# Reordered maxima and wider routing operands in an attention and mixture-of-experts kernel

## The chip, the core and the metric

The kernel runs on one core of a Trainium2 chip. The time is the device time of one execution in microseconds (us); of several executions the median counts. Before the change it is 771.11 us (three runs, 770.67 to 771.77).

A core has a matrix engine (TensorE, PE in the profile; its weight loads are PEld), VectorE (DVE), ScalarE (ACT), GpSimd (POOL), and SyncE (SP), which issues the transfers here. Each engine takes its own instructions strictly in order; between engines there are only semaphores. SBUF is the working memory, PSUM the memory that TensorE writes its products to.

## What is computed

Three layers in a row, all in float32. Inputs have batch 4, 8 heads, 576 tokens of head width 64; the later layers see 2304 rows of 512.

```python
# attention, block-causal with blocks of 64
scores = scale * q @ k.T
scores = where(block_i >= block_j, scores, -1e9)
attn = exp(scores - max(scores)); attn /= sum(attn) + 1e-9
x = attn @ v
# channel mix; x_prev is x one token earlier
xk = mu_k * x + (1 - mu_k) * x_prev;  xr = mu_r * x + (1 - mu_r) * x_prev
x = sigmoid(xr @ w_r) * (relu(xk @ w_k) ** 2 @ w_v)
# one of 8 experts for each token
logits = x @ w_gate
for each token s of a batch row:
    fresh = argmax(logits[s])
    e = fresh if s == 0 or sigmoid(x[s] @ w_local) < 0.5 else previous e
    out[s] = softmax(logits[s])[e] * (relu(x[s] @ w1[e]) @ w2[e])
```

## The kernel before

Products of float32 operands are mostly made of "rounded" parts: an operand is split in a high part (`hi`, the value as float32r) and the rest (`lo`), and the product is the sum of hi x hi, hi x lo and lo x hi. Much of VectorE's, ScalarE's and GpSimd's work is this splitting.

**Attention (0 to about 197 us).** Each of the 32 heads (4 batches of 8) is one round of a loop over `i`, and every engine has that loop written out by hand; the order of the calls in it is the order on the engine. A head has five query tiles of 128 rows, the last with 64 (tiles 0 to 4). The softmax needs each row's maximum before the scores that go to exp are made. Therefore the work is spread over heads: in round `i`

- TensorE makes the masked scores of head `i` in five pieces (`head_scores`, L732 and L733), the products from which the maxima of head `i+2` are read (`head_max`, L707, and L710 for tile 4), the transpose that turns the maxima of head `i+1` into a row (`head_row`, L718), and the value products of head `i` (`head_pv_split`, L774 and L779, and `head_pv_late`, L787 to L789; `head_pv`, L753, in the last four heads). `head_max` has four groups: group 0 is tiles 0 and 1, groups 1, 2, 3 are tiles 2, 3, 4. Groups 0 to 2 wait only at the first of them; group 3 writes to banks of the first two groups and so waits for their maxima (`max_reduced`, count 4i+2).
- VectorE reads the maxima (`head_reduce`, L1380, and L1383 for tile 4), copies the row of L718 (`copy_row`, L1391), casts q and k of head `i+3` (`cast_hi`, L1402), makes the low parts of q (`split_q_lo`, L1407), of the probabilities (`split_p`, L1491), in even rounds of v (`split_v`, L1483 and L1485), and of one piece of the next layer's weights (`split_wm_lo`, L1415, from round 5 on), and inverts the row sums of head `i-1` (`invert`, L1396).
- ScalarE does the exps (L1151), copies of the results out of PSUM (L1175) and the high parts.
- GpSimd makes the low part of k of head `i+3` (`split_k`, L531), which waits for `split_q_lo` of the same head, and multiplies the output of head `i-3` by its inverted sums (`normalise`, L540), which waits for a transfer.

`head_row` of head `i+1` stands in round `i` and waits for all four groups of maxima of that head, of which VectorE takes the last at the end of round `i-1`.

**Channel mix (about 197 to 476 us).** Six steps of 384 tokens, TensorE full with products (`mlp_step`).

**Routing and experts.** While the last two steps run, the routing of the first 12 groups of 128 tokens is worked out (`pre_route`), the remaining 6 follow at 476 to 484 us. Scans along the tokens are done on VectorE, first within a group of 128 (`local`), then over groups (`carry`); transposes and small products on TensorE bring them to the layout needed (`send_local` L853 and L854, `send_carry` L859, `rank_pre` L876, `rank_base` L1025). After that TensorE runs the expert products, 128 tokens a tile.

Of the kernel before, what the change touches and what calls it, by code (L numbers as in the profile page):

```python
# [5 lines left out]
F32 = mybir.dt.float32  # L6
# [3 lines left out]
R32 = mybir.dt.float32r  # L10
# [6 lines left out]
def attention_moe_program(nc, qkT, v, mu_k, mu_r, w_k, w_v, w_r, w_gate9, w1, w2, out):  # L17
# [36 lines left out]
    with ExitStack() as ctx:  # L54
# [138 lines left out]
        keep = place("x", "keep", [G, NG])  # L193
        fresh = place("x", "fresh", [G, NG])
        holds = place("x", "holds", [NG, G])
        local = place("x", "local", [NG, G])
        unset = place("x", "unset", [1, NG])
        carry = place("x", "carry", [1, NG + 2], R32)
        code = r3("code", 1)
        onehot_any = r3("onehot_any", NE, NPRE)  # L200
        onehot_pre = place("x", "onehot_pre", [G, NE, NPRE], R32)
# [3 lines left out]
        cnt_pre = place("x", "cnt_pre", [P, NE])  # L205
        ones_r = place("x", "ones_r", [G, P], R32)
        behind_r = place("x", "behind_r", [G, G], R32)
        base_pre_r = place("x", "base_pre_r", [1, NE, NPRE], R32)
        base_fin_r = place("x", "base_fin_r", [1, NE, NFIN], R32)
        most = place("x", "most", [P, 1])  # L210
        ties = place("x", "ties", [P, NE])
        first_code = place("x", "first_code", [P, 1])
# [477 lines left out]
        def _(pe):  # L690
# [107 lines left out]
            for i in range(NHEAD):  # L798
                ahead = i + 2 < NHEAD
                head_scores(i, (0, 1))  # L800
                if i + 1 < NHEAD:
                    head_row(i + 1)
                if ahead:
                    head_max(i + 2, (0,))
                head_scores(i, (2, 3, 4))
                if ahead:
                    head_max(i + 2, (1,))
                if i < NSPLIT:
                    head_pv_split(i, (0, 1))
                    head_max(i + 2, (2,))  # L810
                    head_pv_split(i, (2, 3, 4, 5))
                    head_max(i + 2, (3,))
                    head_pv_late(i)
                    continue
                head_pv(i, (0, 1))
                if ahead:
                    head_max(i + 2, (2,))
                head_pv(i, (2, 3))
                if ahead:
                    head_max(i + 2, (3,))  # L820
                head_pv(i, (4, 5, 6))
# [28 lines left out]
            def send_local(n, bank, dve_sem, pe_sem):  # L850

                pe.wait_ge(dve_sem, 2)
                nc.tensor.transpose(ps[0:1, bank, P:P + n], local[0:n, G - 1:G], ident[0:n, 0:n])  # L853
                nc.tensor.transpose(ps[0:G, bank, 0:n], local[0:n, :], ident[0:n, 0:n]).then_inc(pe_sem, 1)  # L854

            def send_carry(n, dve_sem, pe_sem):

                pe.wait_ge(dve_sem, 3)
                mm(ps[0:G, 2, 2 * P:2 * P + n], ones_r[0:1, :], carry[:, 0:n], start=True, stop=True).then_inc(pe_sem, 1)  # L859

            def flat(a):

                return a[:, :, :].rearrange("p e g -> p (e g)")
# [6 lines left out]
            def rank_pre():  # L870

                pe.wait_ge(pre_dve, 5)
                dst = ps[0:G, 2, 0:NE * NPRE]
                mm(dst, ones_r[:, :], flat(incl_pre), start=True, stop=False)
                mm(dst, behind_r[:, :], flat(onehot_pre), start=False, stop=False)
                mm(dst, ones_r[0:1, :], flat(base_pre_r), start=False, stop=True).then_inc(pre_pe, 1)  # L876

            def slot_0_pre():

# [142 lines left out]
            def rank_base():  # L1022

                mm(ranks, ones_r[:, :], incl_pre[:, :, NPRE - 1:NPRE].to_broadcast([G, NE, NFIN]), start=True, stop=False)
                mm(ranks, ones_r[0:1, :], flat(base_fin_r), start=False, stop=False)  # L1025

            def rank_fin():

# [340 lines left out]
        def _(dve):  # L1369
# [124 lines left out]
            for i in range(NHEAD):  # L1494
                if i + 1 < NHEAD:
                    copy_row(i + 1)
                if i + 2 < NHEAD:
                    head_reduce(i + 2, 0)
                if i % 2 == 0 and i < NSPLIT:
                    split_v(i // 2)  # L1500
                if WFIRST < i:
                    split_wm_lo(i - 1 - WFIRST)
                if i + NBUF < NHEAD:
                    cast_hi(i + NBUF)
                if i < NSPLIT:
                    split_p(i)
                if i + NBUF < NHEAD:
                    split_q_lo(i + NBUF)
                if i + 2 < NHEAD:
                    head_reduce(i + 2, 1)  # L1510
                    head_reduce(i + 2, 2)
                if i:
                    invert(i - 1)
                if i + 2 < NHEAD:
                    head_reduce(i + 2, 3)
                if i == NHEAD - 3:
                    dve.wait_ge(k_split, NHEAD)
                    dve.wait_ge(q_split, NHEAD)
                if i in (NHEAD - 3, NHEAD - 1):
                    for c in range(2):  # L1520
                        sum_xm(0, 0, c + (i == NHEAD - 1) * 2)
                if i == NHEAD - 2:
                    for c in range(2):
                        xm0_lo(c)
# [5 lines left out]
            def link(ins):  # L1530

                links[0] += 1
                ins.then_inc(chain, 1)
                dve.wait_ge(chain, links[0])
# [100 lines left out]
            def carry_scan(n, bank, pe_sem, dve_sem):  # L1635

                dve.wait_ge(pe_sem, 2)
                link(vec.tensor_scalar(unset[:, 0:n], ps[0:1, bank, P:P + n], 0.0, None, ALU.is_equal))
                vec.tensor_tensor_scan(carry[:, 1:n + 1], unset[:, 0:n], ps[0:1, bank, P:P + n], 0.0,
                                       ALU.mult, ALU.add).then_inc(dve_sem, 1)  # L1640

            def codes(gs, bank, pe_sem):
# [50 lines left out]
            def pre_route(d):  # L1693

                if d == 0:
                    dve.wait_ge(const_done, 3)
                    dve.wait_ge(logits_read, NPRE // GPS)
                    vec.memset(carry[:, 0:1].bitcast(F32), 0.0)
                    vec.tensor_copy(ones_r[:, :], ones_g[:, :])
                    vec.tensor_copy(behind_r[:, :], behind[:, :])  # L1700
                    vec.tensor_copy(base_pre_r[:, :, :], base_pre[:, :, :])
                    vec.tensor_copy(base_fin_r[:, :, :], base_fin[:, :, :])
                    vec.memset(val_1[:, :, 1].bitcast(F32), 0.0)
                    group_tops(pre, pre_dve)
                if d == 1:
                    local_scan(NPRE, pre_pe, pre_dve)
                    carry_scan(NPRE, 3, pre_pe, pre_dve)
                if d == 2:
                    codes(pre, 3, pre_pe)
                    link(vec.tensor_tensor(onehot_any[:, :, :], revs[:, :, pre], over_e(code, pre), ALU.is_equal))  # L1710
                    vec.tensor_reduce(cnt_pre[:, :], onehot_any[:, :, :], AX.X, ALU.add).then_inc(pre_dve, 1)
                if d == 3:
                    first_expert()
                    places(pre, onehot_pre, incl_pre, notfirst_pre, pre_dve)
# [200 lines left out]
```

## Time and profile before

| | |
|---|---|
| median of three runs | 771.11 us |
| the profiled execution | 772.05 us |
| its span, first to last instruction | 770.3 us |
| TensorE busy | 741.0 us, 96% |
| VectorE busy | 494.1 us, 64% |
| ScalarE busy | 357.5 us, 46% |
| GpSimd busy | 182.9 us, 24% |
| mean granted clock of TensorE | 0.991 of full |

Busy shares are averages over stages; between 40 and 170 us VectorE is busy over nine tenths of the time. Of TensorE's clock there are two levels, 1.2 and 2.4 GHz; the profile gives it in parts of the higher. Ends of matrix products are modelled, so two products in a row overlap in the records, and a start is a better mark than an end.

### The profile page before, as it was taken

Reading aid. Unit: us, or ns where it says so; the run is one execution under the profiler, and the core shown is the slowest. Engines: PE = TensorE matmul, PEld = TensorE weight load, DVE = VectorE, ACT = ScalarE, POOL = GpSimd, SP = SyncE. Lnnn points to the kernel's source line nnn. Section 1 sums busy time; section 2 is a strip of 40 time slices with the busy share of each in tenths; the row PEclk is TensorE's granted clock in tenths of the full one; section 3 lists DMA queues with packets and bytes.
Section 4 is the critical chain, followed back from the end, with each engine's and each line's share of the span. In section 5 each row is a group of like instructions: output and inputs, shape, how many; then the busy total and the mean of one; then the engine's idle time right before and its main releaser. Section 6 shows DMA issues by size and latency. Waiting matters only on the chain.

```text
span 770.3 us, 13475 instructions
## 1 busy us (share of the span) xinstructions
PE 741.0 (96%) x4054; PEld 661.7 (86%) x4055; DVE 494.1 (64%) x905; ACT 357.5 (46%) x702; POOL 182.9 (24%) x215
## 2 busy tenths in 40 slices
PE   5999999998999999999999999999999999999994
PEld 4888888886989999999999998788888788888882
DVE  8899999996586856859487797622223745453261
ACT  4687877875652606244251432222124644353250
POOL 3345455453200000000020000223323232323231
PEclk9999999998999999999999999999999999999997
DMA  5667676551000010100101071167110176441000
GB/s 158 212 202 224 195 228 190 165 159 43 24 1 1 0 42 1 42 1 1 42 1 43 3 270 42 43 246 274 41 32 27 41 257 235 143 144 40 20 22 8
DMA packets 43063, 74.41 MB, mean 97 GB/s; under 512 B 10061, under 2 KB 20470, under 8 KB 43012
## 3 DMA queue, kind: packets, MB, share of 16 engines
q1 hardware_dynamic: 38676, 64.30, 25.3%
q0 software_dynamic: 4336, 9.47, 3.6%
q8 instruction: 27, 0.44, 0.2%
q14 instruction: 24, 0.20, 0.1%
HBM read 65.31 MB, written 10.57 MB: 99 GB/s over the span
## 4 chain that ended last, share of the span: by engine, by line
PE 83%; DVE 10%; issue 2%; ACT 2%; DMA 1%; ACTq 0%; POOL 0%; POOLq 0%; DVEq 0%
PE ps L841 20%; PE ps L842 20%; PE ps L843 20%; PE ps L779 3%; PE ps L707 2%; PE ps L999 2%; PE ps L733 2%; PE ps L732 2%; PE ps L831 2%; DVE negm L1380 2%; PE ps L710 2%; PE ps L774 1%; DVE sig L1564 1%; PE ps L753 1%; PE ps L908 1%
## 5 line engine op out<-in xcount | busy, mean ns | idle before, releaser
L841 PE MATMUL ps<-we_hi,hT_hi 128*128 (+1 forms) x176 | 73.4, 417 | 2.1 <-DVE o_sb L1856 1.4
L841 PE MATMUL ps<-we_hi,xgT_hi 128*128 (+1 forms) x176 | 70.6, 401 | 0.2 <-DVE xgT_lo L1755 0.2
L1317 ACT ACTIVATE hT_hi<-ps 128x512 fp32r<-128x512 f32 x44 | 26.1, 597 | 94.5 <-PE ps L999 49.4
L842 PE MATMUL ps<-we_lo,xgT_hi 128*128 (+1 forms) x176 | 69.7, 396 | 0.0
L843 PE MATMUL ps<-we_hi,xgT_lo 128*128 (+1 forms) x176 | 69.7, 396 | 0.0
L842 PE MATMUL ps<-we_lo,hT_hi 128*128 (+1 forms) x176 | 69.5, 395 | 0.0
L843 PE MATMUL ps<-we_hi,hT_lo 128*128 (+1 forms) x176 | 69.4, 394 | 0.0
L1151 ACT ACTIVATE pT<-ps 128x256 f32<-128x256 f32 (+2 forms) x192 | 63.1, 388 | 9.3 <-PE ps L733 8.9
L841 PE MATMUL ps<-xm_k_hi,wk_hi 128*128 128x384 f32 x192 | 65.2, 339 | 2.0 <-DVE ksq L1543 1.7
L841 PE MATMUL ps<-ksq_hi,wv_hi 128*128 128x384 f32 x192 | 66.0, 344 | 0.9 <-DVE yT L1578 0.9
L531 POOL TENSOR_TENSOR hi<-qk_raw,hi 64x576 fp32r<-64x576 f32 x32 | 45.2, 1412 | 85.8 <-DVE aug L1407 85.8
L842 PE MATMUL ps<-ksq_lo,wv_hi 128*128 128x384 f32 x192 | 64.9, 338 | 0.0
L843 PE MATMUL ps<-ksq_hi,wv_lo 128*128 128x384 f32 x192 | 64.9, 338 | 0.0
L843 PE MATMUL ps<-xm_k_hi,wk_lo 128*128 128x384 f32 x192 | 64.6, 336 | 0.0
L842 PE MATMUL ps<-xm_k_lo,wk_hi 128*128 128x384 f32 x192 | 64.5, 336 | 0.0
L1749 DVE TENSOR_TENSOR we_lo<-we_raw,we_hi (+1 forms) x48 | 55.6, 1221 | 11.3 <-ACT we_hi L1296 11.3
L1564 DVE RECIPROCAL sig<-sig 128x384 f32<-128x384 f32 x24 | 61.3, 2553 | 0.8
L1254 ACT ACTIVATE relu_k<-ps 128x384 f32<-128x384 f32 x48 | 23.6, 491 | 81.2 <-PE ps L843 81.2
L1762 DVE TENSOR_TENSOR hT_lo<-ps,hT_hi 128x512 fp32r<-128x512 f32 x44 | 30.0, 686 | 45.2 <-ACT hT_hi L1317 45.2
L1380 DVE TENSOR_REDUCE negm<-ps 128x1 fp32r<-128x128 f32 (+3 forms) x128 | 56.2, 479 | 2.1 <-PE ps L707 0.3
L732 PE MATMUL ps<-hi 128*128 128x256 f32 (+2 forms) x192 | 53.7, 297 | 2.3 <-ACT pT L1151 2.2
L628 POOL DMA_INDIRECT out<-o_sb,idx_out x21 | 21.5, 1023 | 139.4 <-DVE o_sb L1856 139.4
(277 smaller groups left out, 1835.4 us busy)
## 6 DMA issues: line engine op xcount, KB each, us to landing
we_raw<-w SPq DMA_DIRECT2D x12, 2048.0 KB, 11.8
qk_raw<-qkT SPq DMA_DIRECT2D x32, 576.0 KB, 3.9
v_sb<-v SPq DMA_DIRECT2D x16, 320.0 KB, 4.9
inv<-inv_scratch SPq DMA_DIRECT2D x32, 144.0 KB, 4.3
y_scratch<-ytok SPq DMA_DIRECT2D x6, 768.0 KB, 3.5
wk_raw<-w_k SPq DMA_DIRECT2D x8, 256.0 KB, 4.5
wv_raw<-w_v SPq DMA_DIRECT2D x8, 256.0 KB, 4.9
wr_raw<-w_r SPq DMA_DIRECT2D x4, 256.0 KB, 4.8
```

Source lines behind the costliest of these rows:

```text
L531: nc.gpsimd.tensor_tensor(hi[i % NBUF][DH:P, KEY, :], qk_raw[DH:P, i % 2, 1, :], hi[i % NBUF][DH:P, KEY, :].bitcast(F32), ALU.subtract).th ...
L732: mm(dst, hi[b][:, KEY, keys], hi[b][:, Q, q0:q1], start=True, stop=False)
L841: mm(dst, a_hi, b_hi, start=(k == 0), stop=False)
L842: mm(dst, a_hi, b_lo, start=False, stop=False)
L843: return mm(dst, a_lo, b_hi, start=False, stop=(k == n - 1))
L1151: return nc.scalar.activation(dst, src, ACT.Exp, **kw)
L1254: nc.scalar.activation(relu_k[:, f % 2, :], ps[:, KB + f % 2, 0:NT], ACT.Relu).then_inc(relu_done, 1)
L1317: nc.scalar.activation(hT_hi[:, half * FC // 2:(half + 1) * FC // 2, :].rearrange("p f t -> p (f t)"), ps[:, 3 + half, :], ACT.Copy).then_ ...
L1380: last = vec.tensor_reduce(negm[:, i % 2, t:t + 1], ps[:, bank, col:col + keys], AX.X, ALU.max, negate=True)
L1564: vec.reciprocal(sig[:, d, :], sig[:, d, :]).then_inc(sig_done, 1)
L1749: vec.tensor_tensor(we_lo[part][:, third], we_raw[part][:, third], we_hi[part][:, bass.ds(slot_at(j) + k * EPIECE, EPIECE)].bitcast(F32), ...
L1762: vec.tensor_tensor(hT_lo[:, fs, :].rearrange("p f t -> p (f t)"), ps[:, 3 + half, :], hT_hi[:, fs, :].rearrange("p f t -> p (f t)").bitca ...
```

## The change

In the attention loop VectorE's calls stand in another order: the maxima of group 1 (tile 2) directly behind group 0 (and `split_v`), those of group 2 (tile 3) behind `split_p`, and the weight piece behind `split_q_lo`. TensorE makes the product of tile 4 (group 3) between the value products. In the routing, operands that had 1, 12 or 18 rows get 128, of which the rest is zero, and two transposes always take 128 columns.

```diff
@@ placement of tiles
-        local = place("x", "local", [NG, G])
+        local = place("x", "local", [P, G])
-        carry = place("x", "carry", [1, NG + 2], R32)
+        carry = place("x", "carry", [P, NG + 2], R32)
-        base_pre_r = place("x", "base_pre_r", [1, NE, NPRE], R32)
-        base_fin_r = place("x", "base_fin_r", [1, NE, NFIN], R32)
+        base_pre_r = place("x", "base_pre_r", [P, NE, NPRE], R32)
+        base_fin_r = place("x", "base_fin_r", [P, NE, NFIN], R32)
@@ TensorE, the loop over heads
                 if i < NSPLIT:
                     head_pv_split(i, (0, 1))
                     head_max(i + 2, (2,))
-                    head_pv_split(i, (2, 3, 4, 5))
+                    head_pv_split(i, (2, 3))
                     head_max(i + 2, (3,))
+                    head_pv_split(i, (4, 5))
                     head_pv_late(i)
@@ TensorE, routing (send_local; send_carry, rank_pre and rank_base in the same manner)
-                nc.tensor.transpose(ps[0:1, bank, P:P + n], local[0:n, G - 1:G], ident[0:n, 0:n])
-                nc.tensor.transpose(ps[0:G, bank, 0:n], local[0:n, :], ident[0:n, 0:n]).then_inc(pe_sem, 1)
+                nc.tensor.transpose(ps[0:1, bank, P:2 * P], local[:, G - 1:G], ident[:, :])
+                nc.tensor.transpose(ps[0:G, bank, 0:P], local[:, :], ident[:, :]).then_inc(pe_sem, 1)
...
-                mm(ps[0:G, 2, 2 * P:2 * P + n], ones_r[0:1, :], carry[:, 0:n], start=True, stop=True).then_inc(pe_sem, 1)
+                mm(ps[0:G, 2, 2 * P:2 * P + n], ones_r[:, :], carry[:, 0:n], start=True, stop=True).then_inc(pe_sem, 1)
@@ VectorE, the loop over heads
                 if i % 2 == 0 and i < NSPLIT:
                     split_v(i // 2)
-                if WFIRST < i:
-                    split_wm_lo(i - 1 - WFIRST)
+                if i + 2 < NHEAD:
+                    head_reduce(i + 2, 1)
                 if i + NBUF < NHEAD:
                     cast_hi(i + NBUF)
                 if i < NSPLIT:
                     split_p(i)
+                if i + 2 < NHEAD:
+                    head_reduce(i + 2, 2)
                 if i + NBUF < NHEAD:
                     split_q_lo(i + NBUF)
-                if i + 2 < NHEAD:
-                    head_reduce(i + 2, 1)
-                    head_reduce(i + 2, 2)
+                if WFIRST < i:
+                    split_wm_lo(i - 1 - WFIRST)
                 if i:
                     invert(i - 1)
@@ VectorE, pre_route(0)
-                    vec.memset(carry[:, 0:1].bitcast(F32), 0.0)
+                    vec.memset(carry[:, :].bitcast(F32), 0.0)
+                    vec.memset(local[:, :], 0.0)
+                    vec.memset(base_fin_r[:, :, :].bitcast(F32), 0.0)
+                    link(vec.memset(base_pre_r[:, :, :].bitcast(F32), 0.0))
```

How this stands on VectorE in an odd round, from the copy of the row (m_rows) to the maximum of tile 4; "negm" are the maxima, "hi1" the cast q and k, "aug1" takes the low part of q. Before:

```order
L1391 CAST m_rows_76<-ps 5x128 [waits row_loaded0,max_row]
L1380 TENSOR_REDUCE negm_75<-ps 128x1 [waits max_row,max_scores]
L1380 TENSOR_REDUCE negm_75<-ps 128x1
L1415 TENSOR_TENSOR wk_lo_184<-wk_raw_185,wk_hi_179 128x374 [waits wm_is_hi]
L1402 CAST hi1_72<-qk_raw_67 128x1152 [waits qk_loaded0,scores_t]
L1491 TENSOR_TENSOR pT_lo_82<-pT_81,p_hi_83 128x320 [waits p_is_hi]
L1407 TENSOR_TENSOR aug1_73<-qk_raw_67,hi1_72 64x576 [waits hi_cast]
L1380 TENSOR_REDUCE negm_75<-ps 128x1 [waits max_scores] x2
L1396 RECIPROCAL sums_79<-sums_79 64x9 [waits sums_spread0]
L1383 TENSOR_REDUCE negm_75<-ps 64x1 [waits max_scores]
```

And now (lines after the TensorE part are one higher: L1381 is L1380 of before):

```order
L1392 CAST m_rows_76<-ps 5x128 [waits row_loaded0,max_row]
L1381 TENSOR_REDUCE negm_75<-ps 128x1 [waits max_row,max_scores]
L1381 TENSOR_REDUCE negm_75<-ps 128x1
L1381 TENSOR_REDUCE negm_75<-ps 128x1 [waits max_scores]
L1403 CAST hi1_72<-qk_raw_67 128x1152 [waits qk_loaded0,scores_t]
L1492 TENSOR_TENSOR pT_lo_82<-pT_81,p_hi_83 128x320 [waits p_is_hi]
L1381 TENSOR_REDUCE negm_75<-ps 128x1 [waits max_scores]
L1408 TENSOR_TENSOR aug1_73<-qk_raw_67,hi1_72 64x576 [waits hi_cast]
L1416 TENSOR_TENSOR wk_lo_184<-wk_raw_185,wk_hi_179 128x374 [waits wm_is_hi]
L1397 RECIPROCAL sums_79<-sums_79 64x9 [waits sums_spread0]
L1384 TENSOR_REDUCE negm_75<-ps 64x1 [waits max_scores]
```

The maximum of tile 2 (the first row that waits only for `max_scores`) moved up by four instructions, that of tile 3 by one, and the weight piece (wk_lo) moved down past five. In even rounds it is the same with v_hi and v_lo in front of the moved maximum:

```order
L1381 TENSOR_REDUCE negm_75<-ps 128x1 [waits max_row,max_scores]
L1381 TENSOR_REDUCE negm_75<-ps 128x1
L1484 CAST v_hi_84<-v_sb_74 128x128 [waits v_loaded0,pv_done]
L1486 TENSOR_TENSOR v_lo_85<-v_sb_74,v_hi_84 128x128 [waits v_is_hi]
L1381 TENSOR_REDUCE negm_75<-ps 128x1 [waits max_scores]
L1403 CAST hi0_70<-qk_raw_67 128x1152 [waits qk_loaded1,scores_t]
L1492 TENSOR_TENSOR pT_lo_82<-pT_81,p_hi_83 128x320 [waits p_is_hi]
```

On TensorE, between tile 3's product and the late value products (v_hi, pT_lo), in an even round. Before:

```order
L707 MATMUL ps<-aug0_71 128x512
L779 MATMUL ps<-pT_81,v_sb_74 128x320 [waits exp_done,o_copied]
L779 MATMUL ps<-pT_81,v_sb_74 128x320 [waits exp_done]
L779 MATMUL ps<-pT_81,v_sb_74 128x192 [waits exp_done]
L779 MATMUL ps<-pT_81,v_sb_74 128x64 [waits exp_done]
L710 MATMUL ps<-aug0_71 64x288 [waits max_reduced]
L710 MATMUL ps<-aug0_71 64x288
L787 MATMUL ps<-p_hi_83,v_hi_84 128x320 [waits p_split,v_split]
L788 MATMUL ps<-pT_lo_82,v_hi_84 128x320
```

And now:

```order
L707 MATMUL ps<-aug0_71 128x512
L779 MATMUL ps<-pT_81,v_sb_74 128x320 [waits exp_done,o_copied]
L779 MATMUL ps<-pT_81,v_sb_74 128x320 [waits exp_done]
L710 MATMUL ps<-aug0_71 64x288 [waits max_reduced]
L710 MATMUL ps<-aug0_71 64x288
L779 MATMUL ps<-pT_81,v_sb_74 128x192 [waits exp_done]
L779 MATMUL ps<-pT_81,v_sb_74 128x64 [waits exp_done]
L787 MATMUL ps<-p_hi_83,v_hi_84 128x320 [waits p_split,v_split]
L788 MATMUL ps<-pT_lo_82,v_hi_84 128x320
```

The two halves of tile 4's product (L710) moved ahead of the value products of 192 and 64 columns. The product of tile 2, which the moved maximum reads, keeps its place behind the scores.

## Rows read from the trace of the kernel before

**Rows 1.** The page, part 1: busy us, share of the span, instructions.
```profile
PE 741.0 (96%) x4054; PEld 661.7 (86%) x4055; DVE 494.1 (64%) x905; ACT 357.5 (46%) x702; POOL 182.9 (24%) x215
```

**Rows 2.** Timeline, weight loads of L718: start us, length us, engine, line.
```profile
43.20 0.08 PEld L718 LDWEIGHTS ps<-ident_r,negm 128*5 128x5 f32 x1
...
87.80 0.08 PEld L718 LDWEIGHTS ps<-ident_r,negm 128*5 128x5 f32 x1
...
93.19 0.08 PEld L718 LDWEIGHTS ps<-ident_r,negm 128*5 128x5 f32 x1
...
98.97 0.09 PEld L718 LDWEIGHTS ps<-ident_r,negm 128*5 128x5 f32 x1
...
171.49 0.08 PEld L718 LDWEIGHTS ps<-ident_r,negm 128*5 128x5 f32 x1
```

**Rows 3.** Timeline of an odd round (i = 13), same columns, idle time before in brackets.
```profile
88.06 0.28 DVE L1391 CAST m_rows<-ps 5x128 fp32r<-5x128 f32 x1 [0.32 <-PE ps L718]
...
88.41 0.62 DVE L1380 TENSOR_REDUCE negm<-ps 128x1 fp32r<-128x128 f32 x2
...
88.95 0.61 DVE L1415 TENSOR_TENSOR wk_lo<-wk_raw,wk_hi 128x374 fp32r<-128x374 f32 x1
...
89.21 0.42 PE L707 MATMUL ps<-aug 69*128 69x384 f32 x1
...
89.48 0.75 DVE L1402 CAST hi<-qk_raw 128x1152 fp32r<-128x1152 f32 x1
...
90.04 0.48 PE L707 MATMUL ps<-aug 69*128 69x512 f32 x1
...
90.15 0.48 DVE L1491 TENSOR_TENSOR pT_lo<-pT,p_hi 128x320 fp32r<-128x320 f32 x1
...
90.55 0.74 DVE L1407 TENSOR_TENSOR aug<-qk_raw,hi 64x576 fp32r<-64x576 f32 x1
91.22 1.14 DVE L1380 TENSOR_REDUCE negm<-ps 128x1 fp32r<-128x384 f32 x2
...
91.46 1.42 POOL L531 TENSOR_TENSOR hi<-qk_raw,hi 64x576 fp32r<-64x576 f32 x1 [2.31 <-DVE aug L1407]
...
92.29 0.19 DVE L1396 RECIPROCAL sums<-sums 64x9 f32<-64x9 f32 x1
...
92.41 0.73 DVE L1383 TENSOR_REDUCE negm<-ps 64x1 fp32r<-64x576 f32 x1
...
93.09 1.43 POOL L540 TENSOR_TENSOR xT<-o_raw,inv 64x576 f32<-64x576 f32 x1 [0.20 <-POOL hi L531]
```

**Rows 4.** Timeline of the even round behind it, VectorE.
```profile
94.34 0.26 DVE L1483 CAST v_hi<-v_sb 128x128 fp32r<-128x128 f32 x1
...
94.64 0.29 DVE L1485 TENSOR_TENSOR v_lo<-v_sb,v_hi 128x128 fp32r<-128x128 f32 x1
...
94.85 0.54 DVE L1415 TENSOR_TENSOR wk_lo<-wk_raw,wk_hi 128x374 fp32r<-128x374 f32 x1
```

**Rows 5.** Timeline at 15.5 and at 196.4 us, VectorE beside GpSimd.
```profile
15.53 1.40 POOL L531 TENSOR_TENSOR hi<-qk_raw,hi 64x576 fp32r<-64x576 f32 x1 [2.64 <-DVE aug L1407]
...
16.02 1.00 DVE L1483 CAST v_hi<-v_sb 128x128 fp32r<-128x128 f32 x1
...
196.40 1.09 DVE L1469 TENSOR_TENSOR xm_k_lo<-ksq,xm_k_hi 128x384 fp32r<-128x384 f32 x2
...
196.96 1.82 POOL L540 TENSOR_TENSOR xT<-o_raw,inv 64x576 f32<-64x576 f32 x1 [5.43 <-DMA inv<-inv_scratch]
```

**Rows 6.** Timeline at 182 to 186 us, VectorE's sums and TensorE's wait.
```profile
182.22 2.35 DVE L1462 SCALAR_TENSOR_TENSOR ksq<-xT,mu,ksq 128x384 f32<-128x384 f32 x2
...
185.87 0.63 PE L732 MATMUL ps<-hi 128*128 128x320 f32 x1 [2.22 <-ACT pT L1151]
```

**Rows 7.** Windows, 186 to 192: each engine's busy us (instructions), granted clock, transfers.
```profile
186.00:192.00 6.00, 6.00 (x17) 4.64 (x18) 1.53 (x4) 3.32 (x9) 1.40 (x1) 0.50 0.11 27
```

**Rows 8.** Groups by line on TensorE: count, busy us, mean ns, idle before.
```profile
L848 PE MATMUL ps<-idw,fresh 128*12 128x128 f32 (+1 forms) x2 | 0.6, 275 | 0.1
```

More of the change, by code:

```diff
@@ L875, in rank_pre @@
                 mm(dst, behind_r[:, :], flat(onehot_pre), start=False, stop=False)
-                mm(dst, ones_r[0:1, :], flat(base_pre_r), start=False, stop=True).then_inc(pre_pe, 1)
+                mm(dst, ones_r[:, :], flat(base_pre_r), start=False, stop=True).then_inc(pre_pe, 1)
             def slot_0_pre():
@@ L1024, in rank_base @@
                 mm(ranks, ones_r[:, :], incl_pre[:, :, NPRE - 1:NPRE].to_broadcast([G, NE, NFIN]), start=True, stop=False)
-                mm(ranks, ones_r[0:1, :], flat(base_fin_r), start=False, stop=False)
+                mm(ranks, ones_r[:, :], flat(base_fin_r), start=False, stop=False)
             def rank_fin():
@@ L1638, in carry_scan @@
                 link(vec.tensor_scalar(unset[:, 0:n], ps[0:1, bank, P:P + n], 0.0, None, ALU.is_equal))
-                vec.tensor_tensor_scan(carry[:, 1:n + 1], unset[:, 0:n], ps[0:1, bank, P:P + n], 0.0,
+                vec.tensor_tensor_scan(carry[0:1, 1:n + 1], unset[:, 0:n], ps[0:1, bank, P:P + n], 0.0,
                                        ALU.mult, ALU.add).then_inc(dve_sem, 1)
@@ L1697, in pre_route @@
                     dve.wait_ge(logits_read, NPRE // GPS)
-                    vec.memset(carry[:, 0:1].bitcast(F32), 0.0)
+                    vec.memset(carry[:, :].bitcast(F32), 0.0)
+                    vec.memset(local[:, :], 0.0)
+                    vec.memset(base_fin_r[:, :, :].bitcast(F32), 0.0)
+                    link(vec.memset(base_pre_r[:, :, :].bitcast(F32), 0.0))
                     vec.tensor_copy(ones_r[:, :], ones_g[:, :])
                     vec.tensor_copy(behind_r[:, :], behind[:, :])
-                    vec.tensor_copy(base_pre_r[:, :, :], base_pre[:, :, :])
-                    vec.tensor_copy(base_fin_r[:, :, :], base_fin[:, :, :])
+                    vec.tensor_copy(base_pre_r[0:1, :, :], base_pre[:, :, :])
+                    vec.tensor_copy(base_fin_r[0:1, :, :], base_fin[:, :, :])
                     vec.memset(val_1[:, :, 1].bitcast(F32), 0.0)
```

## The prediction

> **What bounds the kernel now.** I read the page first: PE is busy 741.0 of 770.3 us, DVE only 494.1 [rows 1]. That is an average over two stages with different limits, and the change sits in both, so the next view is the timeline of one head of the attention stage. A head runs from one L718 (TensorE transposes the maxima of head i+1, `head_row`) to the next. Its starts give the beat [rows 2]: 87.80 to 93.19 is 5.39 us in an odd round of the loop over i, 93.19 to 98.97 is 5.78 us in an even one, where `split_v` adds two instructions on VectorE. From 43.20 (round 5) to 171.49 (round 28) there are 23 rounds, 12 odd and 11 even, 128.29 us: 12 x 5.39 = 64.68, which leaves 63.61, 5.78 for each even one.
>
> Who sets that beat? In the rows of the odd head [rows 3] VectorE goes from instruction to instruction without idling until its last, the maximum of tile 4 (L1383), which ends at 92.41 + 0.73 = 93.14. L718 waits for just that, and comes at 93.19. Then L1391 copies its product at 93.46, with 0.32 us idle before it, the only gap of the round. So the ring is: L718, VectorE's whole list, L718. TensorE's own stream is nearly as long (it is why the page shows PE full), but the even heads are 0.39 us longer though TensorE does the same work in them: VectorE's list sets them, and the odd ones stand at the tie. The reader should see here that an engine at 64% of the span is the bound of this stage. Anything that VectorE waits for inside its list is therefore paid for, once a head.
>
> **The change, part 1: the maxima of tiles 2 and 3 earlier on VectorE.** No instruction is added or removed in a head; the list is reordered. Measured from L718 (87.80), before: copy 0.26, maxima of tiles 0 and 1 at 0.61, weight piece (L1415) 1.15, cast of q and k (L1402) 1.68, p_lo (L1491) 2.35, q_lo (L1407) 2.75, maxima of tiles 2 and 3 at 3.42, inversion (L1396) 4.49, maximum of tile 4 at 4.61, next L718 at 5.39 [rows 3]. From start to start that is 0.53 for the weight piece, 0.67 the cast, 0.40 p_lo, 0.67 q_lo, 1.07 the two maxima, 0.12 the inversion, 0.78 the last maximum with its handover: 4.24 in sum.
>
> After, the maximum of tile 2 stands straight behind those of tiles 0 and 1. VectorE is there at 1.15. But its operand is the 384-column product of L707, which stands on TensorE behind all scores of the head: it starts at 89.21 and ends at 89.63, 1.83 behind L718 [rows 3], and this place on TensorE is not moved. With 0.05 for the handover (93.14 to 93.19 for the other direction) the maximum starts at 1.88. In an odd round VectorE thus stands idle 0.73 us in the middle of its list, where before the weight piece and the cast covered that time. What is queued behind the waiting instruction is the whole rest, 4.24 us, so the next L718 comes at 1.88 + 4.24 = 6.12 rather than 5.39. The other waits of the new list are met: tile 3's product of 512 columns ends at 90.04 + 0.48 = 90.52, 2.72 behind L718 [rows 3], and VectorE is not at it before 1.88 + 0.67 + 0.40 = 2.95, whatever share tile 2 has. Odd rounds: +0.73.
>
> **Even rounds, and GpSimd.** Here v_hi and v_lo (L1483, L1485) stand in front and fill the gap: before, they take from 94.34 to 94.85, 0.51 [rows 4], so 1.15 + 0.51 = 1.66, and the wait would be only 0.22. But GpSimd moves too. Its `split_k` waits for q_lo: q_lo ends 91.29, split_k starts 91.46 and takes 1.42, `normalise` follows 0.21 later and takes 1.43 [rows 3]. In the new list q_lo starts at 1.88 + 1.07 + 0.67 + 0.40 = 4.02, not 2.75, and the weight piece comes behind it, at 4.69 to 5.23. What happens when both engines want two operands in SBUF: at 16.02 a v_hi cast, otherwise 0.26, takes 1.00 and ends 0.09 behind the end of the GpSimd instruction that was already running (15.53 + 1.40 = 16.93). The other way round, two VectorE subtractions run from 196.40 to 197.49, GpSimd's instruction that starts at 196.96 takes 1.82 instead of 1.42 and ends at 198.78, 1.29 behind VectorE's end [rows 5]. So the later one stands still. For the new list: the weight piece ends at 5.23, split_k at 5.23 + 1.29 = 6.52, normalise runs from 6.73 to 8.16, which is 2.04 behind the next L718 (8.16 - 6.12). In an odd round nothing of VectorE is hit (its cast of q and k starts at 2.35). In an even round v_hi starts at 1.15, inside normalise: it ends at 2.13, v_lo starts at 2.17, the maximum of tile 2 at 2.38, and the head lasts 2.38 + 4.24 = 6.62 instead of 5.78. Even rounds: +0.84. (Before, normalise ended at 94.52 while v_hi began at 94.34, so almost nothing was lost.)
>
> The Trainium skill bears on this place ("SBUF — State Buffer", Terms): VectorE and GpSimd take their common port pair by an exclusive lock for a whole instruction, and the loser blocks rather than shares. Both places above agree. By that rule the even rounds cost what I have here; if the two only shared bandwidth, they would come out as in rival B.
>
> **Rounds 1 to 4** have no weight piece, so their list is 0.53 shorter: 6.12 - 0.53 = 5.59. I take 5.39 for each of them before, as for an odd round: +0.2 each for rounds 1 to 3. Round 4 is even and has the first normalise: 4.93 + 1.42 + 0.21 + 1.42 - 5.59 = 2.39, the maximum at 2.73, the head 2.73 + 3.71 = 6.44, +1.05. Together +1.6 (an estimate from the spacings above).
>
> **Part 2: tile 4's product between value products.** TensorE issues L710 two products sooner. It waits for the maximum of tile 2, which in the new list is done at about 2.4, long before. This removes a wait of a few tenths that even heads show on TensorE. It isn't on the ring: VectorE reads that product last, and arrives there at 5.3, far behind. Worth 0; no more than the 0.39 of an even head if the ring weren't the bound.
>
> **Part 3: routing operands of 128 rows.** Four transposes (L853 and L854, twice) go from 12 or 18 to 128 moving columns. The nearest row is the transpose of 128 columns in the same step, 275 ns [rows 8]; that is 4 x 0.275 = 1.1 as an upper end and 0 as the lower. Most of it is a fixed way through the engine (384 columns in L707 take 0.42 us, 0.15 more for 256 columns, [rows 3]), so 110 columns more are about 0.06 each: 4 x 0.06, rounded up to 0.3. The products with one row have the same columns as before: 0. The memsets and the wait behind them stand on VectorE in the next to last step, while TensorE is full with value products of the MLP: 0. Bounds of the part: 0 and 1.1. I take +0.3.
>
> **The end of attention (rounds 28 to 31).** TensorE waits 2.22 us for an exp, because ScalarE waits for two VectorE sums that take 2.35 together, held up by `normalise` of GpSimd; afterwards the granted clock is 0.50, the 1.2 GHz level, for 6 us [rows 6, 7]. The new order moves both engines by about half a microsecond to one. If the sums come first, up to the 1.4 us of that instruction go, and maybe the low stretch, which costs half of its 6 us: -4.4. Against it, ScalarE waits there for the last split_k, which comes 1.27 later (4.02 - 2.75) and up to 0.3 more: +1.6, and a second low stretch of 3.0 would make +4.6. I take 0 between these ends.
>
> **Sum.** 12 x 0.73 = 8.8; 11 x 0.84 = 9.2; rounds 1 to 4 1.6; routing 0.3; end 0: +19.9. The profiled execution took 772.05 (span 770.3), the median of the runs is 771.11, 0.9 less: 771.11 + 19.9 = 791.0 us.
>
> **Rivals.** A is the forecast. B: the gap in front of tile 2 is there, but v_hi isn't held up by GpSimd (a port that is shared, or a normalise that falls elsewhere, since it also waits for a transfer). Even rounds are then 6.12, +0.34 x 11 = 3.7, with 8.8, 4 x 0.2 and 0.3: +13.6, 784.7 us. Against it the row at 16.02; for it that normalise can come later when its transfer is late, as at 196.96, where GpSimd had waited 5.43 us for one [rows 5].
> C: TensorE's clock. Its stream is 5.39 at most in a head of 6.1 to 6.6, so it idles 0.7 to 1.2 in each. The one fall of this stage came behind 2.22 us of idling [rows 6, 7]; nothing shorter shows one. If the repeated gaps brought one in every fourth head, six stretches of 6 us cost 3 less the slack of a head, about 2 each: +12 on A, 803 us. The Trainium skill ("TensorE: Matmul & The Clock Gate", A second HAM failure mode: psum-queue depth-cycling) tells of just this, short idling between groups of products that makes the clock swing between its levels; no stretch of the heads here shows it yet.
> D, the other side: TensorE, not the ring, sets the heads. Then VectorE's gap is free, the even heads lose their 0.39 x 11 = 4.3, and with the end's -4.4 the time is 762.4; 766.8 without. It decides if L718 could start before VectorE's last maximum ends. Against it: the even heads' 0.39 and the unbroken list.
> E: the reordering changes nothing, since something I don't see covers the gap; with the routing's 0.3, 771.4.
>
> **Chances.** A 0.60, B 0.20, C 0.11, D 0.05, E 0.04. A measurement of this kernel tells about 0.2% (1.5 us) from no change. Faster: D, 0.05. Same: most of E, 0.03. Slower: the rest, 0.92. The range goes from 780 (B with the end at its good bound) to 800 (A with the end and routing at their bad bounds and a little of C); D, E and the most of C lie outside.
>
> **What would show it.** In the profile after: L718 to L718 near 6.1 in odd and 6.6 in even rounds; VectorE idle 0.7 before the maximum of tile 2, put down to L707; TensorE waiting for L1384 (the last maximum, one line later now) before L718; v_hi casts of about 1 us. B is right if these stay at 0.26. C is right if the granted clock is under 1.00 between 20 and 170 us. The forecast is wrong if L718 keeps its 5.39 or if VectorE's idle time turns out not to delay its last maximum.

## The result and the profile after

| | before | after |
|---|---|---|
| median | 771.44 us (4 runs, 770.67 to 773.27) | 789.91 us (4 runs, 788.72 to 791.71) |
| profiled execution | 772.05 us | 791.71 us |
| its span | 770.3 us | 789.9 us |

The ratio is 1.0239, with a 95% interval of 1.0223 to 1.0255: slower by 2.4%. The forecast was 791.0 us.

The page after, part 1 (busy time by engine) and the head of part 4 (the chain of work that ended last):

```profile
PE 744.6 (94%) x4054; PEld 661.4 (84%) x4055; DVE 502.4 (64%) x908; ACT 357.5 (45%) x702; POOL 185.6 (23%) x215
...
PE 72%; DVE 19%; issue 5%; ACT 2%; DMA 1%; ACTq 0%; POOL 0%; POOLq 0%; DVEq 0%
```

Against [rows 1], TensorE is hardly busier (3.6 us more, modelled), yet the span is 19.6 us longer. VectorE's share is still 64%. The share of an engine says nothing here; the chain does, where VectorE now has 19% of the span (10% before).

The weight loads of L718 in the timeline (start us, length us, engine, line, in brackets the idle time before it and who ended it), of rounds 5, 13, 14, 15 and 28, answer to [rows 2]:

```profile
45.42 0.08 PEld L718 LDWEIGHTS ps<-ident_r,negm 128*5 128x5 f32 x1 [0.95 <-DVE negm L1384]
...
95.67 0.08 PEld L718 LDWEIGHTS ps<-ident_r,negm 128*5 128x5 f32 x1 [1.25 <-DVE negm L1384]
...
101.67 0.08 PEld L718 LDWEIGHTS ps<-ident_r,negm 128*5 128x5 f32 x1 [0.68 <-DVE negm L1384]
...
108.23 0.08 PEld L718 LDWEIGHTS ps<-ident_r,negm 128*5 128x5 f32 x1 [1.23 <-DVE negm L1384]
...
189.79 0.08 PEld L718 LDWEIGHTS ps<-ident_r,negm 128*5 128x5 f32 x1 [0.68 <-DVE negm L1384]
```

An odd round (95.67 to 101.67) takes 6.00 us, an even one (101.67 to 108.23) 6.56. From round 5 to round 28 it is 144.37 us instead of 128.29; with 12 odd rounds of 6.00 the even ones are 6.58 on average, the forecast had 6.12 and 6.62. And each L718 now names the one it waited for, the last maximum of VectorE.

The list of waits, TensorE's first and then VectorE's (line waited for: us in total, times, longest):

```profile
PE ps L718 <- DVE negm L1384: 17.7, 26, 1.0
...
PE ps L732 <- ACT pT L1152: 3.0, 2, 1.6
PE ps L710 <- DVE negm L1381: 2.0, 2, 1.5
```

```profile
DVE negm L1381 <- PE ps L707: 14.4, 19, 2.9
```

The first and the last of them were next to nothing before (0.8 us once, and 0.3 us in two waits) and are the two ends of one chain: VectorE waits for tile 2's product, and TensorE waits for VectorE's last maximum. The moved product of tile 4 (L710) waits twice in all (seven times before, 3.0 us in sum), L732 twice at the end of attention.

VectorE's rows of the odd round in the timeline, which answer to [rows 3]:

```profile
96.28 0.62 DVE L1381 TENSOR_REDUCE negm<-ps 128x1 fp32r<-128x128 f32 x2
97.54 0.56 DVE L1381 TENSOR_REDUCE negm<-ps 128x1 fp32r<-128x384 f32 x1 [0.64 <-PE ps L707]
98.02 0.75 DVE L1403 CAST hi<-qk_raw 128x1152 fp32r<-128x1152 f32 x1
...
99.08 0.68 DVE L1381 TENSOR_REDUCE negm<-ps 128x1 fp32r<-128x512 f32 x1
...
100.35 0.53 DVE L1416 TENSOR_TENSOR wk_lo<-wk_raw,wk_hi 128x374 fp32r<-128x374 f32 x1
100.81 0.20 DVE L1397 RECIPROCAL sums<-sums 64x9 f32<-64x9 f32 x1
100.93 0.69 DVE L1384 TENSOR_REDUCE negm<-ps 64x1 fp32r<-64x576 f32 x1
```

L718 stood at 95.67. The maximum of tile 2 starts at 97.54, 1.87 behind it, with 0.64 us idle in front (forecast 1.88). From there to the next L718 at 101.67 it is 4.13 us. The forecast said 4.24: it had added up spacings of before in which the weight piece was stretched by the end of a GpSimd instruction (0.53 from start to start; here 0.46) and the last maximum took 0.78 to L718 (here 0.74).

GpSimd beside VectorE in the even round behind it, which answers to [rows 4]. First GpSimd, then VectorE:

```profile
100.59 1.56 POOL L531 TENSOR_TENSOR hi<-qk_raw,hi 64x576 fp32r<-64x576 f32 x1 [2.84 <-DVE aug L1408]
102.36 1.41 POOL L540 TENSOR_TENSOR xT<-o_raw,inv 64x576 f32<-64x576 f32 x1 [0.20 <-POOL hi L531]
```

```profile
102.83 1.04 DVE L1484 CAST v_hi<-v_sb 128x128 fp32r<-128x128 f32 x1
103.90 0.29 DVE L1486 TENSOR_TENSOR v_lo<-v_sb,v_hi 128x128 fp32r<-128x128 f32 x1
104.11 0.55 DVE L1381 TENSOR_REDUCE negm<-ps 128x1 fp32r<-128x384 f32 x1
```

split_k takes 1.56 instead of 1.42, because the weight piece (100.35 to 100.88) holds the port that both need when it wants to start; it ends at 102.15, 6.48 behind L718 (forecast 6.52). normalise ends at 103.77, and v_hi, at the port since 102.83, takes 1.04 instead of 0.26 and ends at 103.87. Without that, v_hi and v_lo would be through by 103.34 and tile 2's maximum would start at 1.87 again, at 103.54; it starts at 104.11. That is the 0.56 us by which an even round is longer than an odd one. No run took v_hi off VectorE in the changed kernel; this step is read from the rows.

The chain that ended last shows the same in order of time (start us, us, what):

```profile
95.67 0.23 PE ps L718
...
97.25 0.27 PE ps L707
...
98.02 0.75 DVE hi L1403
...
101.01 0.62 DVE negm L1384
...
101.68 0.23 PE ps L718
```

Before, that chain ran through TensorE's products alone in an odd round (87.80 to 93.19); in an even one it went over VectorE's list as far as tile 2's maximum and back to TensorE by L710. Now it leaves TensorE behind tile 2's product (L707) and stays on VectorE until L718: read downward, it is the ring of the prediction.

### The profile page after: what moved, and what is told of

The parts are those of the page before. It is cut to its first block, busy times and chain, and to the rows that moved or that the text cites. A ratio compares the mean times of both kernels' runs of the same rounds, so it can differ in the third digit from the quotient of the medians.

```text
span 789.9 us, 13478 instructions
## 1 busy us (share of the span) xinstructions
PE 744.6 (94%) x4054; PEld 661.4 (84%) x4055; DVE 502.4 (64%) x908; ACT 357.5 (45%) x702; POOL 185.6 (23%) x215
## 4 chain that ended last, share of the span: by engine, by line
PE 72%; DVE 19%; issue 5%; ACT 2%; DMA 1%; ACTq 0%; POOL 0%; POOLq 0%; DVEq 0%
PE ps L842 19%; PE ps L844 19%; PE ps L843 19%; DVE negm L1381 3%; DVE sig L1566 3%; PE ps L1000 2%; DVE hi L1403 2%; PE ps L707 2%; DVE negm L1384 2%; PE ps L832 2%; PE ps L733 2%; PE ps L732 2%; DVE aug L1408 1%; DVE v_hi L1484 1%; PE ps L909 1%
## 5 line engine op out<-in xcount | busy, mean ns | idle before, releaser
L531 POOL TENSOR_TENSOR hi<-qk_raw,hi 64x576 fp32r<-64x576 f32 x32 | 48.8, 1526 | 102.0 <-DVE aug L1408 102.0
L1381 DVE TENSOR_REDUCE negm<-ps 128x1 fp32r<-128x128 f32 (+3 forms) x128 | 59.1, 485 | 16.1 <-PE ps L707 14.4
L1318 ACT ACTIVATE hT_hi<-ps 128x512 fp32r<-128x512 f32 x44 | 26.1, 597 | 94.5 <-PE ps L1000 49.4
L732 PE MATMUL ps<-hi 128*128 128x256 f32 (+2 forms) x192 | 53.5, 296 | 3.0 <-ACT pT L1152 3.0
```

Source lines behind the costliest of these rows:

```text
L531: nc.gpsimd.tensor_tensor(hi[i % NBUF][DH:P, KEY, :], qk_raw[DH:P, i % 2, 1, :], hi[i % NBUF][DH:P, KEY, :].bitcast(F32), ALU.subtract).th ...
L732: mm(dst, hi[b][:, KEY, keys], hi[b][:, Q, q0:q1], start=True, stop=False)
L1318: nc.scalar.activation(hT_hi[:, half * FC // 2:(half + 1) * FC // 2, :].rearrange("p f t -> p (f t)"), ps[:, 3 + half, :], ACT.Copy).then_ ...
L1381: last = vec.tensor_reduce(negm[:, i % 2, t:t + 1], ps[:, bank, col:col + keys], AX.X, ALU.max, negate=True)
```

## Experiments

All medians are set against the same kernel before, run on the same chip: 771.39 us for the first four, 771.43 for the last four.

### VectorE's order alone

Only the calls on VectorE in the attention loop are in the new order; TensorE's loop and the routing are as before.

```diff
+                if i + 2 < NHEAD:
+                    head_reduce(i + 2, 1)
                 if i + NBUF < NHEAD:
                     cast_hi(i + NBUF)
...
+                if WFIRST < i:
+                    split_wm_lo(i - 1 - WFIRST)
```

> Only VectorE's order in the attention loop is changed. Theory (ring of L718 and VectorE's list: idle time before tile 2's maximum, GpSimd blocks v_hi): this part carries everything, rounds of 6.0 and 6.6 us, 789.5 us. Rival (the cost comes from TensorE's moved product of tile 4 or from the routing): 771 to 775 us.

Measured: 789.83 us, ratio 1.0243 (1.0204 to 1.0282). L718 comes every 6.00 us in odd and 6.56 in even rounds, as in the whole change (789.91), and TensorE waits for VectorE's last maximum as there:

```profile
PE ps L718 <- DVE negm L1383: 18.6, 25, 1.1
```

This part carries all of the loss; the rival is out.

### TensorE's order alone

```diff
-                    head_pv_split(i, (2, 3, 4, 5))
+                    head_pv_split(i, (2, 3))
                     head_max(i + 2, (3,))
+                    head_pv_split(i, (4, 5))
```

> Only TensorE's order: tile 4's product stands before the value products of 192 and 64 columns, VectorE as before. Theory: with VectorE's old order the maximum of tile 2 ends about 3.9 us behind L718 in an odd round and 4.3 in an even one, while TensorE now reaches the waiting product at 3.7; TensorE stands and has 1.73 us of work from there to the next L718, so odd rounds grow to 5.7 and even ones to 6.1 us: about +7, 778.5 us. Rival (that product is off the ring in either order, as the prediction had it for the whole change): within 1 us of 771.4.

Measured: 781.10 us, ratio 1.0121 (1.0086 to 1.0156). Rounds take 5.73 and 6.18 us. VectorE's two maxima and L710 in an even round, then L710 in an odd one:

```profile
103.27 1.14 DVE L1381 TENSOR_REDUCE negm<-ps 128x1 fp32r<-128x384 f32 x2
...
103.86 0.47 PE L710 MATMUL ps<-aug 69*64 69x288 f32 x2 [0.61 <-DVE negm L1381]
...
109.59 0.48 PE L710 MATMUL ps<-aug 69*64 69x288 f32 x2 [0.17 <-DVE negm L1381]
```

L710 waits for the first of the two maxima (tile 2, whose half of the 1.14 us is the first) and starts as it ends. In sum:

```profile
PE ps L710 <- DVE negm L1381: 11.4, 29, 1.5
```

That is 29 waits; with VectorE's new order there are two (the waits of the changed kernel, above), and the kernel before had seven. So the moved product costs 9.7 us by itself and nothing in the company of the earlier maximum. Its price depends on the other part, and prices of single parts don't add up: 18.4 for VectorE's order and 9.7 for TensorE's, 18.5 together. The forecast's 0 for it was right only for the change as a whole. The median is 2.6 us above the theory's 778.5 (which the interval, +6.6 to +12.0 us, still holds): that had counted only rounds from 5 on, and rounds 1 to 4 take 5.73 too (1.1 us in the profiled executions); from round 5 on, rounds of 5.73 and 6.18 cost about 1.5 us more than those of 5.7 and 6.1 that it had.

### Routing operands of 128 rows alone

```diff
-                nc.tensor.transpose(ps[0:G, bank, 0:n], local[0:n, :], ident[0:n, 0:n]).then_inc(pe_sem, 1)
+                nc.tensor.transpose(ps[0:G, bank, 0:P], local[:, :], ident[:, :]).then_inc(pe_sem, 1)
...
```

> Only the routing operands of 128 rows. Theory: four transposes a little longer, +0.3 us, 771.7 us. Rival: the memsets and transposes reach TensorE, +1 us or more, 772.5 us.

Measured: 771.22 us, ratio 0.9990 (0.9972 to 1.0008): no change that can be told. In the changed kernel the transposes show as follows (count, busy us, mean ns, idle before):

```profile
L855 PE MATMUL ps<-idw,local 128*128 128x128 f32 x2 | 0.5, 271 | 0.0
```

In the mean 271 ns: about what the transpose of 128 columns had, 275 [rows 8]. Before, with 12 and 18 columns, it took 209 ns, and the other transpose (L853, now L854) went from 170 to 271. For the four that is 0.33 us, as the forecast's 0.3 says, and less than these runs resolve.

### The weight piece back in front of tile 2's maximum

In the changed kernel, VectorE's idle time of 0.64 us would hold the weight piece (0.53). It looks like the repair:

```diff
+                if WFIRST < i:
+                    split_wm_lo(i - 1 - WFIRST)
                 if i + 2 < NHEAD:
                     head_reduce(i + 2, 1)
...
-                if WFIRST < i:
-                    split_wm_lo(i - 1 - WFIRST)
```

> The changed kernel, with the weight piece (split_wm_lo) put back in front of tile 2's maximum, where it could fill VectorE's idle time. Theory with GpSimd's exclusive port: normalise now ends about 2.46 us behind L718 and holds up the weight piece too, odd rounds 6.4, even 6.9 us, about +9 on the changed kernel: 798.7 us. Rival (only the idle time counts, the port doesn't matter): odd 5.5, even 5.8 us, 775 us.

Measured: 797.65 us, ratio 1.0336 (1.0298 to 1.0374), with odd rounds of 6.40 and even ones of 6.85. An odd round:

```profile
98.09 0.08 PEld L718 LDWEIGHTS ps<-ident_r,negm 128*5 128x5 f32 x1 [0.96 <-DVE negm L1384]
...
99.08 1.41 POOL L540 TENSOR_TENSOR xT<-o_raw,inv 64x576 f32<-64x576 f32 x1 [0.20 <-POOL hi L531]
...
99.25 1.65 DVE L1416 TENSOR_TENSOR wk_lo<-wk_raw,wk_hi 128x374 fp32r<-128x374 f32 x1
...
104.49 0.08 PEld L718 LDWEIGHTS ps<-ident_r,negm 128*5 128x5 f32 x1 [0.97 <-DVE negm L1384]
```

normalise runs until 100.49; the weight piece, begun at 99.25, takes 1.65 us instead of 0.54 and ends at 100.90. Filling the gap with an instruction that needs the port made it 7.7 us slower than the changed kernel (789.91). The rival, by which only the idle time counts, is off by 23 us. So the port is a cost of its own beside the idle time, and here the one that decides.

### Tile 2's product early too

```diff
                 if ahead:
-                    head_max(i + 2, (0,))
+                    head_max(i + 2, (0, 1))
                 head_scores(i, (2, 3, 4))
-                if ahead:
-                    head_max(i + 2, (1,))
```

> The changed kernel, with TensorE's product for tile 2 also moved: it stands with that of tiles 0 and 1, ahead of the scores of 448, 320, 192 and 64 columns. VectorE's idle time before that maximum must go. Theory with GpSimd's port: normalise ends 2.1 us behind L718, so in odd rounds the cast of q and k, which now starts at 1.63, is held up by 0.47 and a round takes 5.75; in even rounds v_hi is held up as before, 6.57. Together -3 on the changed kernel, 786.5 us. Rival (the idle time is all that costs): odd 5.4, even 5.8 us, 772 us.

Measured: 784.42 us, ratio 1.0174 (1.0157 to 1.0190). Rounds: odd 5.62, even 6.57. In the odd round from 92.89 to 98.52:

```profile
93.50 1.09 DVE L1379 TENSOR_REDUCE negm<-ps 128x1 fp32r<-128x128 f32 x3
93.57 1.42 POOL L540 TENSOR_TENSOR xT<-o_raw,inv 64x576 f32<-64x576 f32 x1 [0.20 <-POOL hi L531]
...
94.69 0.92 DVE L1401 CAST hi<-qk_raw 128x1152 fp32r<-128x1152 f32 x1
...
98.52 0.08 PEld L718 LDWEIGHTS ps<-ident_r,negm 128*5 128x5 f32 x1 [0.29 <-DVE negm L1382]
```

VectorE has no idle time before tile 2's maximum any more (three maxima in a row, 93.50 to 94.59). Now the cast of q and k is what meets normalise (until 94.99) and takes 0.92 instead of 0.75. The theory had the mechanism but took the cast to begin at 1.63; it begins at 1.80, so only 0.17 is lost to the port and not 0.47. Even rounds are as predicted, since v_hi meets normalise as before. The rival's 772 would have needed even rounds of 5.8. So taking the idle time away gave back 5.5 of the 18.5 us: in even rounds it had lain behind v_hi's wait for GpSimd and cost nothing of its own.

### v_hi on ScalarE, in the kernel before

```diff
@@ ScalarE, head_exp
+                    if i % 2 == 0 and i < NSPLIT and j == 1:
+                        act.wait_ge(v_loaded[i // 2 % 2], 16 * (i // 4) + 16)
+                        nc.scalar.activation(v_hi[:, DH:3 * DH], v_sb[:, i // 2 % 2, 0, DH:3 * DH], ACT.Copy).then_inc(v_is_hi, 1)
@@ VectorE, split_v
-                vec.tensor_copy(v_hi[:, mine], v_sb[:, j % 2, 0, mine]).then_inc(v_is_hi, 1)
```

> The kernel before, with the cast v_hi on ScalarE, between its second and third exp of an even round. Theory (VectorE's list sets the even rounds): they lose 0.27 us, 5.78 to 5.51, -3.0 in 11 rounds: 768.3 us. Rival (ScalarE's 0.3 us delays an exp that TensorE waits for): 771 us or more.

Measured: 769.20 us, ratio 0.9965 (0.9950 to 0.9979). In the even round from 93.17 on:

```profile
93.82 0.32 ACT L1167 ACTIVATE v_hi<-v_sb 128x128 fp32r<-128x128 f32 x1
...
97.37 0.19 PEld L710 LDWEIGHTS ps<-aug 69*64 69x64 f32 x2
...
98.70 0.08 PEld L718 LDWEIGHTS ps<-ident_r,negm 128*5 128x5 f32 x1
```

The even round takes 98.70 - 93.17 = 5.53 us instead of 5.78, 0.25 less for 0.27 us of work taken off VectorE. So VectorE's list did set the even rounds of the kernel before, at 64% busy, as the prediction read. But it set them only as far as tile 2's maximum, and there the prediction was wrong: it closed the ring at the last maximum and put L710 off it. L710 in the kernel before, in the odd round from 87.80 and the even one from 93.19:

```profile
91.87 0.20 PEld L710 LDWEIGHTS ps<-aug 69*64 69x64 f32 x2
...
97.64 0.19 PEld L710 LDWEIGHTS ps<-aug 69*64 69x64 f32 x2 [0.30 <-DVE negm L1380]
```

It comes 4.07 us behind L718 in the odd round and 4.45 in the even one, where it waits for tile 2's maximum. From L710 to the next L718 it is 1.32 to 1.33 us in every round from 5 to 27, odd or even. All of the 0.39 us by which an even round was longer is lost in front of L710; with v_hi on ScalarE it comes at 97.37, 4.20 behind. The gain is 2.2 us by the medians, 1.6 to 3.9 by the interval, which holds the 3.0 expected.

### The two high parts one round later, in the kernel before

```diff
@@ ScalarE, the loop over heads
+                if i == NHEAD - 2:
+                    for c in range(2):
+                        xm0_hi(c)
                 copy_out(i, 0)
-                if i == NHEAD - 3:
-                    for c in range(2):
-                        xm0_hi(c)
```

> The kernel before, with ScalarE's first two high parts for the channel mix made one round later, behind the exps of head 30 instead of ahead of them. Theory for the end of attention: TensorE's wait of 2.2 us before head 30's exp goes and with it the stretch at granted clock 0.50 that follows (3 us): -4.5, 766.8 us. Rival (the low clock comes from something else, or the channel mix starts later for it): -1.5 at most, 770 us.

Measured: 768.53 us, ratio 0.9964 (0.9955 to 0.9973). The product that had waited for the exps of head 30, then the granted clock (the number after the engines' busy times):

```profile
185.57 0.35 PE L732 MATMUL ps<-hi 128*128 128x320 f32 x1
```

```profile
184.00:190.00 6.00, 5.45 (x34) 4.60 (x33) 4.88 (x9) 5.02 (x14) 1.42 (x1) 1.00 0.10 29
```

The wait of 2.22 us [rows 6] is gone and the granted clock stays 1.00, the 2.4 GHz level, where [rows 7] had 0.50. In its profile the stretch from round 28 to the first product of the channel mix is

```profile
173.54 0.08 PEld L718 LDWEIGHTS ps<-ident_r,negm 128*5 128x5 f32 x1
...
194.82 0.41 PE L841 MATMUL ps<-xm_k_hi,wk_hi 128*128 128x384 f32 x1 [0.26 <-DVE xm_k_lo L1469]
```

194.82 - 173.54 = 21.28 us, against 197.64 - 171.49 = 26.15 in the profile of before: -4.9, near the theory's -4.5. The medians show only -2.9, by the interval -3.5 to -2.1, which holds neither the theory's -4.5 nor the rival's -1.5. The profiled execution of before was not a typical one. The kernel with only the routing changed has the same attention loop and the same wait (2.16 us) before head 30's exp; but in its profile the low clock lasts about 3.4 us, against 6.8 before, and this stretch takes 24.60 us, 3.3 more than here. How long the clock stays low behind one and the same wait differs from execution to execution, and the theory's 3 us for it were too many. In two other kernels such a wait (2.14 us with TensorE's order alone, 2.23 with VectorE's) left the clock at 1.00. That the wait alone brings the low clock is therefore not shown; that the kernel gets faster without it is.

### All three parts for a faster kernel

The kernel before with v_hi on ScalarE, the two high parts later, and on VectorE

```diff
-                if i:
-                    invert(i - 1)
                 if i + 2 < NHEAD:
                     head_reduce(i + 2, 3)
+                if i:
+                    invert(i - 1)
```

> The kernel before, with v_hi on ScalarE, the inversion of the sums behind tile 4's maximum (it fills VectorE's wait for L718), and the two high parts later. Theory: even rounds at TensorE's own 5.39 (-0.39 in 11 rounds, -4.3), end of attention -4.5: 762.6 us. Rival (the parts cover the same loss, or TensorE has another limit at 5.5): 767 us.

Measured: 765.64 us, ratio 0.9931 (0.9917 to 0.9946), 5.8 us faster than before and the fastest here. It is 3 us short of the theory, whose 762.6 lies outside the interval, and nearer to the rival. About half of that is the end of attention, taken at -4.5 where the run above measured -2.9. The other half: even rounds take 5.52 us and not 5.39. The trace says why (even round from 93.00, odd from 98.52):

```profile
93.00 0.08 PEld L718 LDWEIGHTS ps<-ident_r,negm 128*5 128x5 f32 x1
...
96.60 1.14 DVE L1383 TENSOR_REDUCE negm<-ps 128x1 fp32r<-128x384 f32 x2
...
97.20 0.19 PEld L710 LDWEIGHTS ps<-aug 69*64 69x64 f32 x2
...
98.52 0.08 PEld L718 LDWEIGHTS ps<-ident_r,negm 128*5 128x5 f32 x1
...
102.59 0.20 PEld L710 LDWEIGHTS ps<-aug 69*64 69x64 f32 x2
```

TensorE does the same work from L718 to L710 in both. In the even round L710 loads its weights at 97.20, 4.20 behind L718; in the odd one at 102.59, 4.07 behind. Before it in the even round stands tile 2's maximum, the first of the two from 96.60. From L710 to L718 it is 1.32 and 1.33. This is the ring of the kernel before over tile 2's maximum and L710, the one that the experiment on TensorE's order had lengthened: the inversion moved off the wait for L718 doesn't help where L710 waits for tile 2. I had left this ring out of the 5.39.

## Why the prediction was right

By its own steps, in us of the profiled executions (span 789.9 - 770.3 = 19.6):

| step | forecast | measured |
|---|---|---|
| odd rounds 5 to 27, 12 of them | +8.8 | +7.3 |
| even rounds 6 to 26, 11 of them | +9.2 | +8.8 |
| rounds 1 to 4 | +1.6 | +1.3 |
| round 0 | not priced | +0.9 |
| end of attention, round 28 to the channel mix | 0 (-4.4 to +4.6) | +1.3 |
| routing, channel mix and experts | +0.3 | 0.0 |
| sum | +19.9 | +19.6 |

- **What sets the head**: in the changed kernel the ring of L718 and VectorE's whole list, as forecast. Shown by the 26 waits of L718 after. For the kernel before the reading was half right: in even rounds VectorE's list was the bound, but over tile 2's maximum and L710, which the prediction called off the ring (the runs with v_hi on ScalarE and with TensorE's order alone). The sum did not suffer, because the new order makes that ring the shorter one: in the changed kernel L710 comes 3.36 us behind L718, and from it to the next L718 it is 2.6 us in odd rounds and 3.2 in even ones.
- **The idle time before tile 2's maximum**: 1.87 behind L718, forecast 1.88. Right. The remaining list is 4.13, not 4.24; that is the whole difference of 1.5 us in the odd rounds.
- **GpSimd's port**: normalise's end behind the next L718 was forecast at 2.04; it is 103.77 - 101.67 = 2.10. v_hi takes 1.04 us. The run with the weight piece in front, which was expected to lose 9 us and lost 7.7, bears this out.
- **The moved product of tile 4 at 0**: right in the changed kernel, and wrong as a statement about that edit alone (+9.7) and about the ring of before.
- **Routing at 0.3**: the four transposes take 0.33 us longer in the rows; in the runs' times it is below what they resolve. The upper end of 1.1 was wide.
- **Round 0** is 8.35 instead of 7.40 us. It isn't the change: it was 8.29 with only the routing changed and 9.10 in the run with the high parts later, where VectorE's and TensorE's first rounds are those of before. Part of the agreement of the totals to 0.3 us is therefore luck. The profiled execution of after is also the slowest of its four: by the medians the change costs 18.5 us where the forecast had 19.9, about what the odd rounds were priced too high.

The end of attention: ScalarE did wait for the last split_k, 1.4 us longer than before (0.8), priced at +1.6. The row with its idle time of 2.17, and the windows of TensorE behind it, with the granted clock third from the end:

```profile
195.98 1.12 ACT L1206 ACTIVATE ksq<-xT,omu 128x384 f32<-128x384 f32 x2 [2.17 <-POOL hi L531]
```

```profile
196.00:200.00 4.00, 2.61 (x12) 2.14 (x11) 1.01 (x4) 3.81 (x10) 2.80 (x2) 0.76 0.04 6
...
209.00:212.00 3.00, 3.00 (x9) 2.04 (x9) 1.02 (x3) 1.48 (x3) 0.92 (x1) 0.55 0.16 53
```

TensorE waited twice for an exp there (3.0 us in sum, 1.6 the longest) and there are two low stretches; the sum is +1.3. The bounds held, and the middle was a guess, no more. Much of it belongs to the single executions: with VectorE's order alone TensorE waited 1.40 and 2.23 us there, the granted clock stayed at 1.00, and the end took 24.4 us, against 27.5 here and 26.1 before.

Of the rivals, B falls by v_hi's 1.04 us. C falls: TensorE waits up to 1.0 us in a head (17.7 us in 26 waits), and yet the granted clock over all the heads is 1.00:

```profile
20.00:190.00 170.00, 153.39 (x935) 132.30 (x935) 148.48 (x321) 121.17 (x297) 76.80 (x52) 1.00 0.57 177
```

The Trainium skill's warning ("TensorE: Matmul & The Clock Gate", A second HAM failure mode: psum-queue depth-cycling) doesn't show at this spacing. What the prediction said under C, that nothing shorter than 2.22 us of idling shows a fall, no longer holds: the first low stretch above came behind a wait of 1.39. D and E fall by the rounds of 6.00 and 6.56.

## What to carry to other kernels

Look for the ring, not for the busy share: if an engine's instruction list never idles between two handovers to and from another engine, each wait put inside that list can cost its full length per turn (here 0.64 us idle, rounds 0.61 longer), however low the engine's share of the span. Before an instruction is moved forward, find on the producing engine where its operand is made; taking a maximum "sooner" than its product only moves the wait to the front of the queue. And when VectorE's work is reordered, draw GpSimd's two-input instructions beside it: whatever releases them decides which VectorE instructions they will block, and a gap is only worth filling with work that doesn't need their common port.

## What was not expected of the hardware

GpSimd's side of the port was priced from one row, and holds everywhere: split_k, held up by VectorE's weight piece in 24 of 32 rounds, took 1.53 to 1.60 us in them and 1526 ns in the mean of all 32, instead of 1412. The blocked VectorE instruction ends at a fixed distance behind GpSimd's end, 0.13 to 0.16 us less than it takes undisturbed: 0.10 us for v_hi (103.77 to 103.87; undisturbed 0.26), 0.41 for the weight piece (100.49 to 100.90; 0.54) and 0.62 for the cast of q and k (94.99 to 95.61; 0.75). What it has already waited doesn't matter: in the kernel before, the weight piece of 88.95 met the last 0.20 us of a normalise that ended at 89.15, and ended at 89.56, 0.41 behind too. Reading maxima from PSUM and the short inversion run beside GpSimd untouched: the inversion at 100.81 takes 0.20 us while split_k is under way. And the granted clock does not follow from the length of one wait. At the end of attention it fell behind waits of 1.4 and 1.6 us in the changed kernel, and stayed at 1.00 behind waits of 1.40 and 2.23 us with VectorE's order alone and of 2.14 us with TensorE's; behind the 26 waits of up to 1.0 us in the heads it never fell. What decides it stays open.
